# An attention and two gated layers on one core: the prologue before the first token block rebuilt

## The chip, the cores and the metric

The kernel runs on one core of a Trainium2 chip. TensorE (PE) multiplies matrices into PSUM, VectorE (DVE) and ScalarE (ACT) do elementwise work, GpSimd (POOL) does elementwise work on SBUF, SyncE (SP) issues most of the loads and stores. The engines run side by side and meet at semaphores. The metric is the time of one execution on the device in microseconds (us), and lower is better.

## What is computed

q, k and v have 6016 rows and 256 columns. The columns of q and k are normalised, their product is a 256 x 256 matrix of scores, its softmax is applied to v, and two token-wise layers follow.

```python
qn = q / (np.linalg.norm(q, axis=1, keepdims=True) + 1e-06)
kn = k / (np.linalg.norm(k, axis=1, keepdims=True) + 1e-06)
s = kn.transpose(0, 2, 1) @ qn / tau
a = np.exp(s - s.max(-1, keepdims=True))
a /= a.sum(-1, keepdims=True) + 1e-09
x = v @ a                                    # 6016 x 256
h = x @ w_in                                 # 6016 x 2048
P = a[0] + a[1] * h + a[2] * h**2 + a[3] * h**3
Q = 1.0 + np.abs(b[0]) * np.abs(h) + np.abs(b[1]) * h**2
y = (P / (Q + 1e-6)) @ w_out                 # 6016 x 256
out = (sigmoid(y @ w_gate) * (y @ w_val)) @ moe2_w_out   # hidden width 1536
```

In P, a is the input of four coefficients, elsewhere the softmax.

## The kernel before

**The prologue.** k and q come in 14 chunks of 1, 2, 4 x 10, 2 and 2 row tiles, through a ring of three buffers in `work` that SP fills (L277 to L285). PE adds each chunk's product into the scores (L658, fp32, two records for each 256-column product). ACT squares each chunk (L373, L376) and DVE adds the squares (L520). When all is added, DVE folds the sums (L509) and PE turns them into column norms (L665, L667). ACT takes the roots (L383, L384), DVE inverts them and scales the scores in two halves `c` (L526 to L536), finds the maximum of both halves in one instruction (L538) and negates it (L539). ACT takes the exponentials (L389), PE transposes them (L673), DVE copies the transposes to `att_t` (L545). PE then multiplies `att_t` by w_in into M, the product of softmax and w_in, in ten tiles in fp32 (`m_tile`, L648): four 256 columns wide ahead of block 0, the other six 512 wide, one in each of slots 0 to 5 of block 0. ACT and DVE split each tile into a high and a low part in fp32r (`split_m`, L363 and L486).

**Products in three.** All later products are of split operands, three fp32r matmuls for each (high by high, high by low, low by high; `product3`, L637 to L639, and `add_y`, L705 to L707). The weights are split too, in 13 chunks of 128 x 1024: ACT writes the high part (`weights_hi`, L351), POOL the low part (`weights_lo`, L327). Chunks 0 to 3 are w_out of the first layer, 4 to 9 the gate and value weights, 10 to 12 the last weights. Chunks 0 to 3 are split in the loads of k and q, 4 to 7 around the M tiles, 8 to 12 at the slots of the table `SPLIT`.

**The blocks.** The tokens are taken in 16 blocks of 376, each in 8 slots `j`, one slot for two of the 16 column tiles of h. In a slot PE multiplies v's block by M (`hidden`, twelve matmuls). ACT reads the result out of PSUM twice (L430, L433; the second signals `h_read`). DVE multiplies on (L598, L604: the Horner steps `horner1` and `horner2`), and both build the quotient P/Q by a seed and one Newton step: L448, L620 (`quad`), L462 (`seed`), then for the pair of the slot before L584, L588 (`scaled`), L414, L558 and L565 (`g`). Two slots later ACT splits the quotient's high part (L441) and POOL its low part (L339), and three slots later `add_y` multiplies it by w_out, twelve matmuls. PE's `hidden` waits for the slot before's L604 (`horner2`), since both use the same PSUM banks. The next token block's v is split by ACT and DVE (`split_v`, L357 and L480) at the head of its block, after the last `hidden` of the block before. The gate, value and last products of block 0 start in slot 3 of block 1, and from there on each slot has work of both layers.

Each engine runs its instructions in the order in which the code writes them. Names of code in what follows: `g_ready` is signalled by L565, `w_hi_ready` by L351, `w_lo_ready` by L327, `v_lo_ready` by L480, `norms_summed` by the norm matmuls.

Of the kernel before, what the change touches and what calls it, by code (L numbers as in the profile page):

```python
# [17 lines left out]
P = 128  # L18


def attention_rational_gated_kernel(nc, q, k, v, tau, w_in, w_out1, coef_a, coef_b, w_gate, w_val, w_out2, out):
# [39 lines left out]
    KQ_SPLIT = {4: 0, 6: 1, 8: 2, 10: 3}  # L61
    M_SPLIT = ((4, 5), (6, 7))
    KQ_SPLITS, READY = len(KQ_SPLIT), 8
    SPLIT = {(0, 0): 8, (0, 1): 9, (0, 6): 10, (0, 7): 11, (1, 0): 12}
    KQ_T = 4
    KQ_SIZES = [1, 2] + [KQ_T] * ((NT - 5) // KQ_T)
    KQ_SIZES += [2] * ((NT - sum(KQ_SIZES)) // 2) + [1] * ((NT - sum(KQ_SIZES)) % 2)
    KQ_CHUNKS = [(sum(KQ_SIZES[:n]), w) for n, w in enumerate(KQ_SIZES)]
    assert sum(KQ_SIZES) == NT and KQ_SIZES[-1] <= 2
    KQ_RING = 3  # L70

    with ExitStack() as ctx:
# [8 lines left out]
        w_stages = CC * C, 8 * TB  # L81
        with nc.sbuf_tensor("before", [P, 8 * TB + 8 * TB + CC * FF1], F32) as before:
            att_t = before[:, 0:CC * C].rearrange("p (a b) -> p a b", a=CC)
            early_stages = [before[:, at + n * W_CHUNK:at + (n + 1) * W_CHUNK]
                            for at in w_stages for n in range(2)]

            w_in_sb = [before[:, 16 * TB + d * FF1:16 * TB + (d + 1) * FF1] for d in range(CC)]
# [5 lines left out]
        w2_hi, w2_lo = sb("w2_hi", [P, T2, C], F32R), sb("w2_lo", [P, T2, C], F32R)  # L93


# [8 lines left out]
        KQ_W = KQ_T * C  # L104
        work = sb("work", [P, 10 * KQ_W])
# [15 lines left out]
        V_AT = 9 * PW  # L121
        v_in = region(V_AT, (CC, TB))
        STAGE_AT = V_AT + PW
        o_sb = region(STAGE_AT, (CC, TB))
        sg = [region(STAGE_AT + PW + n * TB, (TB,)) for n in range(2)]
        assert STAGE_AT + 2 * PW <= 10 * KQ_W
# [670 lines left out]
```

## Time and profile before

| | us |
|---|---|
| median of 3 runs | 1247.23 |
| the three runs | 1246.74 to 1249.14 |
| the profiled execution | 1247.94 |
| its span, first to last instruction | 1246.4 |
| first matmul of the scores | 4.63 |
| first `hidden` of block 0 | 66.25 |
| first `hidden` of slot 3 of block 1 | 158.50 |

The span is 1.5 us less than the profiled execution's own time, and that is 0.7 us above the median. In a row of the profile "ps<-v_hi,m_hi" means that the instruction writes `ps` and reads `v_hi` and `m_hi`; an arrow in brackets names what ended an engine's idle time. Matmul records overlap: one record of 0.33 us is followed 0.17 us later by the next where PE runs freely.

### The profile page before, as it was taken

How to read it: one execution, taken by the hardware profiler on the slowest of the kernel's cores; microseconds unless marked ns; L12 is line 12 of the kernel's file. 1: busy time of each engine (PE TensorE's matmuls, PEld its weight loads, DVE VectorE, ACT ScalarE, POOL GpSimd, SP SyncE). 2: the span in 40 equal slices, each digit the busy share in tenths (PEclk: the TensorE clock that was granted, in tenths of full speed). 3: DMA queues.
4: the chain of work that ended last, by engine and by line, in shares of the span. 5: the costliest groups of instructions: out<-in, count | busy, mean ns of one | idle time of the engine just before them, and what ended most of it. 6: DMA issues, size and time to landing. Idle time of an engine off the chain costs nothing.

```text
span 1246.4 us, 19492 instructions
## 1 busy us (share of the span) xinstructions
PE 1195.6 (96%) x6766; PEld 1175.9 (94%) x6766; DVE 1084.2 (87%) x1372; ACT 886.5 (71%) x1264; POOL 269.1 (22%) x150
## 2 busy tenths in 40 slices
PE   8768599999999999999999999999999999999998
PEld 6656599999999999999999999999999999999998
DVE  5779898989999998989999998989999998989842
ACT  5667577867777777867777777767777777767732
POOL 1252421212212222212212212212221212212210
PEclk9889799999999999999999999999999999999999
DMA  8820000000000000000000000000000000000000
GB/s 309 315 84 1 12 2 13 14 13 12 0 12 12 12 12 12 12 12 12 0 12 12 12 12 12 12 12 12 0 12 12 12 12 12 12 0 12 0 13 13
DMA packets 14708, 33.82 MB, mean 27 GB/s; under 512 B 1632, under 2 KB 5472, under 8 KB 14432
## 3 DMA queue, kind: packets, MB, share of 16 engines
q1 hardware_dynamic: 14256, 33.56, 7.7%
q8 instruction: 11, 0.18, 0.1%
q14 instruction: 9, 0.07, 0.0%
q10 hardware_dynamic: 432, 0.00, 0.0%
HBM read 27.40 MB, written 6.16 MB: 27 GB/s over the span
## 4 chain that ended last, share of the span: by engine, by line
PE 90%; DVE 5%; ACT 2%; issue 2%; DMA 1%; SPq 0%; DVEq 0%; ACTq 0%
PE ps L637 17%; PE ps L639 17%; PE ps L638 17%; PE ps L705 7%; PE ps L706 7%; PE ps L707 7%; PE ps L729 5%; PE ps L731 5%; PE ps L730 5%; PE ps L658 2%; DMA work<-in_q 1%; DVE work L620 1%; DVE work L598 1%; ACT work L433 1%; PE ps L648 1%
## 5 line engine op out<-in xcount | busy, mean ns | idle before, releaser
L339 POOL TENSOR_TENSOR g_parts<-work,g_parts 128x752 fp32r<-128x752 f32 x128 | 234.1, 1829 | 856.2 <-ACT g_parts L441 850.2
L430 ACT ACTIVATE work<-ps,neg_a 128x752 f32<-128x752 f32 x128 | 125.4, 979 | 155.7 <-PE ps L639 92.1
L637 PE MATMUL ps<-v_hi,m_hi 128*128 128x376 f32 x512 | 175.0, 342 | 31.5 <-DVE work L604 15.5
L639 PE MATMUL ps<-v_hi,m_lo 128*128 128x376 f32 x512 | 174.8, 341 | 0.0
L638 PE MATMUL ps<-v_lo,m_hi 128*128 128x376 f32 x512 | 173.8, 339 | 0.0
L705 PE MATMUL ps<-g_parts,w_hi 128*128 128x376 f32 x512 | 172.9, 338 | 0.0
L706 PE MATMUL ps<-g_parts,w_hi 128*128 128x376 f32 x512 | 170.9, 334 | 0.0
L707 PE MATMUL ps<-g_parts,w_lo 128*128 128x376 f32 x512 | 170.2, 332 | 0.0
L598 DVE TENSOR_TENSOR work<-work,ps 128x752 f32<-128x752 f32 x128 | 119.6, 934 | 47.3 <-ACT work L433 45.5
L462 ACT ACTIVATE work<-work,consts 128x752 f32<-128x752 int32 x128 | 117.6, 919 | 52.6 <-DVE work L620 52.6
L553 DVE TENSOR_TENSOR work<-work,ps 128x376 f32<-128x376 f32 x192 | 103.9, 541 | 52.6 <-PE ps L639 39.9
L414 ACT ACTIVATE work<-work,consts 128x752 f32<-128x752 f32 x128 | 118.3, 924 | 27.9 <-DVE work L584 27.9
L565 DVE SCALAR_TENSOR_TENSOR work<-work 128x752 f32<-128x752 f32 x128 | 122.2, 954 | 14.2
L637 PEld LDWEIGHTS ps<-v_hi,m_hi 128*128 128x128 f32 x512 | 98.4, 192 | 36.4 <-issue 14.2
L620 DVE TENSOR_TENSOR work<-work 128x752 f32<-128x752 f32 x128 | 132.2, 1032 | 0.0
L588 DVE SCALAR_TENSOR_TENSOR work<-work,neg_a 128x752 f32<-128x752 f32 x128 | 131.7, 1029 | 0.0
L409 ACT ACTIVATE ys<-work 128x376 fp32r<-128x376 f32 x192 | 98.9, 515 | 46.0 <-PE ps L731 45.9
L448 ACT ACTIVATE work<-work,abs_b 128x752 f32<-128x752 f32 x128 | 130.6, 1020 | 0.0
L604 DVE SCALAR_TENSOR_TENSOR work<-work,neg_a,ps 128x752 f32<-128x752 f32 x128 | 127.5, 996 | 2.9
L729 PE MATMUL ps<-ys,w_hi 128*128 128x376 f32 x384 | 129.1, 336 | 0.2 <-DVE ys L571 0.2
L637 PE MATMUL ps<-ys,wg_hi 128*128 128x376 f32 x384 | 127.9, 333 | 1.2 <-DVE ys L614 0.8
L639 PE MATMUL ps<-ys,wv_lo 128*128 128x376 f32 x384 | 128.7, 335 | 0.0
(94 smaller groups left out, 2869.2 us busy)
## 6 DMA issues: line engine op xcount, KB each, us to landing
work<-in_v SPq DMA_DIRECT2D x16, 376.0 KB, 3.0
out<-work SPq DMA_DIRECT2D x16, 376.0 KB, 2.3
work<-in_k SPq DMA_DIRECT2D x10, 512.0 KB, 4.7
work<-in_q SPq DMA_DIRECT2D x10, 512.0 KB, 6.1
before<-in_moe_w_out SPq DMA_DIRECT2D x6, 512.0 KB, 6.1
before<-in_moe_w_in SPq DMA_DIRECT2D x2, 1024.0 KB, 6.7
before<-in_moe_w_gate SPq DMA_DIRECT2D x3, 512.0 KB, 7.2
work<-in_moe_w_val SPq DMA_DIRECT2D x2, 512.0 KB, 10.1
```

The source lines that it names most:

```text
L339: nc.gpsimd.tensor_tensor(g_lo[n], g[n], as_f32(g_hi[n]), ALU.subtract).then_inc(g_lo_ready, 1)
L448: nc.scalar.activation(vb, ab, ACT.Identity, scale=abs_b[:, 1:2], bias=abs_b[:, 0:1]).then_inc(vb_ready, 1)
L588: nc.vector.scalar_tensor_tensor(out=poly[o], in0=poly[o], scalar=neg_a[:, 0:1], in1=seed[o], op0=ALU.add, op1=ALU.mult).then_inc(scaled, 1)
L598: nc.vector.tensor_tensor(poly[n], poly[n], ps_h, ALU.mult).then_inc(horner1, 1)
L620: nc.vector.tensor_tensor(quad[n], vb, ab, ALU.mult).then_inc(quad_ready, 1)
L637: nc.tensor.matmul(dst, l_hi, r_hi, start=(n == 0), stop=False)
L638: nc.tensor.matmul(dst, l_hi, r_lo, start=False, stop=False)
L639: last = nc.tensor.matmul(dst, l_lo, r_hi, start=False, stop=(n == len(parts) - 1))
L705: nc.tensor.matmul(acc_y[:, c, :], l_hi, r_hi, start=(j == 0 and x == 0), stop=False)
L706: nc.tensor.matmul(acc_y[:, c, :], l_hi, r_lo, start=False, stop=False)
L707: last = nc.tensor.matmul(acc_y[:, c, :], l_lo, r_hi, start=False, stop=(j == PAIRS - 1 and x == 1))
L729: nc.tensor.matmul(acc_o[:, c, :], l_hi, s_hi[n], start=(m == 0), stop=False)
```

## The change

It touches only what runs before block 1's slot 3, and the waits that go with it.

- **Two load queues.** The q half of the first four chunks is issued by ACT, the k half by SP. The small coefficient loads move behind chunk 3, and the DVE instructions on them behind chunk 6. The chunks are 1, 1, 2, 4 x 10 and 3 tiles, the ring has four buffers, in a place of its own (`kq`). v's block 0 is loaded after chunk 5, two of w_out's chunks after chunks 4 and 6, the other two and w_in (in eight pieces) behind the last chunk.
- **Norms amid the scores.** PE runs the norm matmuls ahead of the last chunk's products. ACT takes the q root first, then the k root, then splits w_out's chunks 2 and 3.
- **Softmax by halves.** For each half c: scores, minimum (of negated scores; the separate negation goes), exponential, transpose into a bank of its own, copy. `split_v(0)` moves ahead of the roots.
- **Block 0's y in fp32.** For block 0's pairs PE multiplies the unsplit quotient `g` by w_out as loaded (`w1_raw`): four fp32 matmuls (`add_raw_y`) instead of twelve fp32r ones, one slot earlier. ACT's and POOL's splits of `g` (L441, L339) fall away for these eight pairs.
- **Splits placed by slot.** Chunk 4's high part is done before block 0, those of 5 to 12 at the ends of slots 0 to 7; the low part of chunk 4 + n waits on POOL for `h_read` of slot n.
- **`split_v(1)`** moves from the head of block 1 to slot 7 of block 0.

```diff
+    KQ_SIZES = [1, 1, 2] + [4] * ((NT - 4) // 4) + [(NT - 4) % 4] * ((NT - 4) % 4 > 0)
+    KQ_RING = 4
+    V_AFTER, COEF_AFTER = 5, 3
+    W1_AFTER = {4: 0, 6: 1}
+    NORMS_BEFORE = len(KQ_CHUNKS) - 1
...
         def splits_v(i, first):
-            return first and not is_block(i, 0)
+            return first and not is_block(i, 0) and not is_block(i, 1)
...
+                if n >= KQ_RING:
+                    sp.dma_start(q_in[r][:, 0:w * C], q_v[:, t * C:(t + w) * C]).then_inc(kq_loaded[r], 16)
...
-            for n in range(READY):
+            for n in range(W1_CHUNKS):
                 weights_lo(n)
             def step(i, first, carry, head, tail):
                 for j, now, late, old, gone, early, second, left in slots(i, first, carry, head, tail):
-                    if old is not None:
+                    if isinstance(i, int) and i * PAIRS + j < len(chunks) - W1_CHUNKS:
+                        pool.wait_ge(h_read, now + 1)
+                        weights_lo(W1_CHUNKS + now)
+                    if old is not None and not unsplit(old):
...
+            split_v(0)
             act.wait_ge(consts_ready, 1)
             nc.scalar.activation(consts[:, 2:3], consts[:, 1:2], ACT.Sqrt, scale=-1.0)
             act.wait_ge(norms_summed, 1)
-            act.wait_ge(kq_multiplied, len(KQ_CHUNKS))
-            nc.scalar.activation(k_norm, ps_knorm, ACT.Sqrt)
             nc.scalar.activation(q_inv, ps_qnorm, ACT.Sqrt).then_inc(norms_rooted, 1)
+            nc.scalar.activation(k_norm, ps_knorm, ACT.Sqrt).then_inc(norms_rooted, 1)
+            for n in range(len(W1_AFTER), W1_CHUNKS):
+                weights_hi(n)
             nc.scalar.activation(consts[:, 3:4], consts[:, 1:2], ACT.Exp)
...
+            link(nc.vector.tensor_scalar(q_inv, q_inv, 1e-6, None, ALU.add))
+            link(nc.vector.reciprocal(q_inv, q_inv))
+            dve.wait_ge(norms_rooted, 2)
+            link(nc.vector.tensor_scalar(k_norm, k_norm, 1e-6, None, ALU.add))
             link(nc.vector.reciprocal(k_inv, k_norm))
             link(nc.vector.tensor_scalar(k_inv, k_inv, tau_inv, None, ALU.mult))
+            dve.wait_ge(kq_multiplied, len(KQ_CHUNKS))
             for c in range(CC):
                 link(nc.vector.scalar_tensor_tensor(out=att[:, c, :], in0=ps_kq[:, c, :], scalar=k_inv[:, c:c + 1],
                                                     in1=q_inv, op0=ALU.mult, op1=ALU.mult))
-            link(nc.vector.reduce_max(neg_max, att, AX_X))
-            nc.vector.tensor_scalar(neg_max, neg_max, -1.0, None, ALU.mult).then_inc(scores_ready, 1)
-            split_v(0)
+                nc.vector.tensor_reduce(neg_min[:, c:c + 1], att[:, c, :], AX_X, ALU.min).then_inc(scores_ready, 1)
+            for c in range(CC):
+                dve.wait_ge(att_turned, c + 1)
+                nc.vector.tensor_copy(att_t[:, :, c * P:(c + 1) * P], ps_attt[c]).then_inc(att_t_ready, 1)
...
+            def add_raw_y(pair):
+                j, n = pair % PAIRS, pair % 2
+                pe.wait_ge(g_ready, pair + 1)
+                for c in range(CC):
+                    for x in range(2):
+                        last = nc.tensor.matmul(acc_y[:, c, :], w1_raw[:, 2 * j + x, c * P:(c + 1) * P], g[n][:, x, :],
+                                                start=(j == 0 and x == 0), stop=(j == PAIRS - 1 and x == 1))
+                last.then_inc(y_added, 1)
...
+                    if old is not None and unsplit(old):
+                        add_raw_y(old)
```

ACT between the last squares and the first M tiles, before (L380 loads the roots' function table, L385 the exponential's, L391 the sigmoid's):

```order
L380 ACT_TABLE_LOAD
L380 ACTIVATE consts<-consts 128x1 [waits consts_ready]
L383 ACTIVATE small<-ps 128x2 [waits kq_multiplied,norms_summed]
L384 ACTIVATE work<-ps 128x256
L385 ACT_TABLE_LOAD
L385 ACTIVATE consts<-consts 128x1
L357 ACTIVATE v_hi<-work 128x752 [waits v_loaded]
L389 ACTIVATE work,small<-work,small 128x256 [waits scores_ready]
L389 ACTIVATE work,small<-work,small 128x256
```

The same place with the change (L366 is `weights_hi`):

```order
L372 ACTIVATE v_hi<-work 128x752 [waits v_loaded]
L401 ACT_TABLE_LOAD
L401 ACTIVATE consts<-consts 128x1 [waits consts_ready]
L403 ACTIVATE work<-ps 128x256 [waits norms_summed]
L404 ACTIVATE small<-ps 128x2
L366 ACTIVATE w_hi<-before 128x1024 [waits w_loaded2]
L366 ACTIVATE w_hi<-before 128x1024 [waits w_loaded3]
L407 ACT_TABLE_LOAD
L407 ACTIVATE consts<-consts 128x1
L410 ACTIVATE work,small<-work,small 128x256 [waits scores_ready] x2
```

Two weight splits now stand between the roots and the exponentials, POOL's low parts follow them, and the roots no longer wait for the last product of the scores.

POOL's splits in block 0, before:

```order
L339 TENSOR_TENSOR g_parts<-work,g_parts 128x752 [waits g_hi_ready] x2
L339 TENSOR_TENSOR g_parts<-work,g_parts 128x752 [waits y_added,g_hi_ready] x3
L327 TENSOR_TENSOR w_lo<-before,w_hi 128x1024 [waits w_hi_ready]
L339 TENSOR_TENSOR g_parts<-work,g_parts 128x752 [waits y_added,g_hi_ready]
L327 TENSOR_TENSOR w_lo<-before,w_hi 128x1024 [waits w_hi_ready]
```

And with the change:

```order
L338 TENSOR_TENSOR wg_lo<-before,wg_hi 128x2x512 [waits w_hi_ready,h_read]
L338 TENSOR_TENSOR wv_lo<-before,wv_hi 128x2x512 [waits w_hi_ready,h_read]
L338 TENSOR_TENSOR wg_lo<-before,wg_hi 128x2x512 [waits w_hi_ready,h_read]
L338 TENSOR_TENSOR wv_lo<-work,wv_hi 128x2x512 [waits w_hi_ready,h_read]
L338 TENSOR_TENSOR wg_lo<-work,wg_hi 128x2x512 [waits w_hi_ready,h_read]
```

Each slot has one weight split there now, and none of the quotient.

DVE at the end of block 0, before (from `horner2` of slot 7):

```order
L604 SCALAR_TENSOR_TENSOR work<-work,neg_a,ps 128x752 [waits horner1]
L620 TENSOR_TENSOR work<-work 128x752 [waits e2_ready,vb_ready]
L558 SCALAR_TENSOR_TENSOR work<-work 128x752 [waits scaled]
L565 SCALAR_TENSOR_TENSOR work<-work 128x752 [waits newton1,e2_ready]
L480 TENSOR_TENSOR v_lo<-work,v_hi 128x752 [waits v_hi_ready]
```

With the change:

```order
L621 SCALAR_TENSOR_TENSOR work<-work,neg_a,ps 128x752 [waits horner1]
L502 TENSOR_TENSOR v_lo<-work,v_hi 128x752 [waits v_hi_ready]
L639 TENSOR_TENSOR work<-work 128x752 [waits e2_ready,vb_ready]
L575 SCALAR_TENSOR_TENSOR work<-work 128x752 [waits scaled]
L582 SCALAR_TENSOR_TENSOR work<-work 128x752 [waits newton1,e2_ready]
```

The split of v's block 1 moved ahead of three instructions.

## Rows read from the trace of the kernel before

**Rows 1.** Busy time by stretches, then TensorE's granted clock, DMA share, GB/s.

```profile
130.00:140.00 10.00, 4.14 (x13) 4.14 (x14) 8.59 (x8) 3.51 (x4) 2.34 (x1) 0.50 0.14 39
...
160.00:200.00 40.00, 39.61 (x231) 39.23 (x230) 37.87 (x50) 30.64 (x44) 9.08 (x5) 1.00 0.00 1
...
300.00:1200.00 900.00, 900.00 (x5244) 899.73 (x5243) 818.43 (x1048) 663.42 (x957) 187.66 (x103) 1.00 0.03 10
```

**Rows 2.** Timeline (start, us, engine, line), slot 3 of block 1 on PE.

```profile
158.50 0.41 PE L637 MATMUL ps<-v_hi,m_hi 128*128 128x376 f32 x1 [1.95 <-DVE work L604]
```

**Rows 3.** Timeline, PE, the product of the scores, in stretches.

```profile
4.63 2.07 PE L658 MATMUL ps<-work 128*128 128x256 f32 x4 [4.63 <-DMA work<-in_q]
8.13 41.93 PE L658 MATMUL ps<-work 128*128 128x256 f32 x184 [1.42 <-DMA work<-in_q]
...
11.64 4.70 PE L658 MATMUL ps<-work 128*128 128x256 f32 x21
```

**Rows 4.** Timeline, from the norms to the maximum.

```profile
51.94 0.68 PE L667 MATMUL ps<-work,ones 128*128 128x256 f32 x2
...
52.72 0.38 ACT L384 ACTIVATE work<-ps 128x256 f32<-128x256 f32 x1
...
53.46 1.75 DVE L530 RECIPROCAL work<-work 128x256 f32<-128x256 f32 x1
...
55.53 1.00 DVE L536 SCALAR_TENSOR_TENSOR work<-ps,small,work 128x256 f32<-128x256 f32 x2
56.57 0.69 DVE L538 TENSOR_REDUCE small<-work 128x2 f32<-128x512 f32 x1
```

**Rows 5.** Timeline, from the exponentials to block 0.

```profile
57.50 0.51 ACT L389 ACTIVATE work<-work,small 128x256 f32<-128x256 f32 x1 [2.17 <-DVE small L539]
...
59.37 0.69 DVE L545 COPY before<-ps 128x512 f32<-128x512 f32 x1 [0.37 <-PE ps L673]
...
60.11 6.49 PE L648 MATMUL ps<-before 128*128 128x256 f32 x16 [0.78 <-DVE before L545]
...
66.25 0.52 PE L637 MATMUL ps<-v_hi,m_hi 128*128 128x376 f32 x1
```

**Rows 6.** Weight splits on POOL (a group, one alone), two DVE instructions beside such splits.

```profile
L327 POOL TENSOR_TENSOR wg_lo<-before,wg_hi 128x1024 fp32r<-128x1024 f32 x3 | 7.0, 2349 | 18.8 <-ACT wg_hi L351 18.8
...
83.69 2.98 POOL L327 TENSOR_TENSOR wv_lo<-work,wv_hi 128x1024 fp32r<-128x1024 f32 x1 [4.57 <-ACT wv_hi L351]
...
84.38 3.09 DVE L588 SCALAR_TENSOR_TENSOR work<-work,neg_a 128x752 f32<-128x752 f32 x1
...
133.34 2.46 DVE L480 TENSOR_TENSOR v_lo<-work,v_hi 128x752 fp32r<-128x752 f32 x1 [0.75 <-ACT v_hi L357]
```

**Rows 7.** Timeline, POOL and then DVE in slot 4 of block 0.

```profile
104.22 1.80 POOL L339 TENSOR_TENSOR g_parts<-work,g_parts 128x752 fp32r<-128x752 f32 x1 [5.84 <-ACT g_parts L441]
...
103.86 1.00 DVE L604 SCALAR_TENSOR_TENSOR work<-work,neg_a,ps 128x752 f32<-128x752 f32 x1
104.77 0.74 DVE L486 SCALAR_TENSOR_TENSOR m_lo<-ps,small,m_hi 128x512 fp32r<-128x512 f32 x1
105.43 1.39 DVE L620 TENSOR_TENSOR work<-work 128x752 f32<-128x752 f32 x1
106.74 0.93 DVE L558 SCALAR_TENSOR_TENSOR work<-work 128x752 f32<-128x752 f32 x1
...
111.49 1.00 DVE L604 SCALAR_TENSOR_TENSOR work<-work,neg_a,ps 128x752 f32<-128x752 f32 x1
```

**Rows 8.** ACT: the second read of h in slot 5, and the weights' high parts (a group).

```profile
109.70 0.79 ACT L433 ACTIVATE work<-ps 128x752 f32<-128x752 f32 x1
...
L351 ACT ACTIVATE w_hi<-before 128x1024 fp32r<-128x1024 f32 x6 | 6.3, 1042 | 0.0
```

**Rows 9.** Timeline, PE: an M tile of 512 columns, and slot 0 of block 1.

```profile
76.33 1.88 PE L648 MATMUL ps<-before 128*128 128x512 f32 x4
...
135.86 0.68 PE L637 MATMUL ps<-v_hi,m_hi 128*128 128x376 f32 x1 [10.57 <-DVE v_lo L480]
```

More of the change, by code:

```diff
@@ L103, in attention_rational_gated_kernel @@
         PW = 2 * TB
[L104 to L105 removed]
+        STAGE_AT = 10 * PW
+        work = sb("work", [P, STAGE_AT + 2 * W_CHUNK])
         def region(at, shape):
@@ L228, in is_block, with unsplit @@
             return isinstance(i, int) and i == n
+        def unsplit(pair):
+            return isinstance(pair, int) and pair < PAIRS
         def splits_v(i, first):
-            return first and not is_block(i, 0)
+            return first and not is_block(i, 0) and not is_block(i, 1)
         def steps(eng, step):
@@ L396, in _ @@
                 split_m(n)
-            for n in M_SPLIT[1]:
-                weights_hi(n)
+            weights_hi(W1_CHUNKS)
             act.wait_ge(coefs_ready, 1)
@@ L435, in step @@
                         split_m(M_FIRST + j)
-                    if old is not None:
+                    if is_block(i, 0) and j == PAIRS - 1:
+                        split_v(1)
+                    if old is not None and not unsplit(old):
                         act.wait_ge(g_ready, old + 1)
+                        if is_block(i, 1):
+                            act.wait_ge(y_added, PAIRS)
+                            act.wait_ge(w_lo_ready, len(chunks))
                         wait_count(act, y_added, old + (-1))
-                        if is_block(i, 0) and j == 2:
-                            act.wait_ge(w_lo_ready, READY)
                         nc.scalar.activation(g_hi[n], g[n], ACT.Copy).then_inc(g_hi_ready, 1)
@@ L460, in step @@
                         act.wait_ge(quad_ready, now + 1)
-                        wait_count(act, g_lo_ready, now + (-1))
+                        if unsplit(now) or (is_block(i, 1) and j < 2):
+                            wait_count(act, y_added, now + (-1))
+                        else:
+                            act.wait_ge(g_lo_ready, now + (-1))
                         nc.scalar.activation(seed[n], quad[n].bitcast(I32), ACT.Sigmoid, scale=SEED_SCALE,
@@ L525, in _ @@
-            dve.wait_ge(norms_rooted, 1)
-            nc.vector.tensor_scalar(q_inv, q_inv, 1e-6, None, ALU.add).then_inc(small_step, 1)
-            nc.vector.tensor_scalar(k_norm, k_norm, 1e-6, None, ALU.add).then_inc(small_step, 1)
-            done[0] += 2
-            dve.wait_ge(small_step, done[0] - 1)
-            nc.vector.reciprocal(q_inv, q_inv).then_inc(small_step, 1)
-            dve.wait_ge(small_step, done[0])
-            done[0] += 1
+                if n == COEF_AFTER + 3:
+                    constants()
@@ L611, in step @@
                         split_m(M_FIRST + j)
+                    if is_block(i, 0) and j == PAIRS - 1:
+                        split_v(1)
                     if j == 2 and head:
@@ L755, in step @@
                         gate_and_value(*early)
-                    if gone is not None:
+                    if gone is not None and not unsplit(gone):
                         add_y((j - 3) % PAIRS, gone, i)
```

196 lines of the change are left out of this document (98 added, 98 removed).

## The prediction, made before the changed kernel ran

> **What bounds the kernel now.** I read the stretches first. From 160 us on PE is busy all the time at full clock (900.00 of 900 us between 300 and 1200) [rows 1], so from there the time is PE's work, which the change leaves as it is. Ahead of that PE waits: of the ten us from 130 on it works 4.14, at the lower clock level (granted 0.50, 1.2 GHz). The timeline shows where this ends: `hidden` of slot 3 of block 1 starts at 158.50 after a wait for DVE's L604 [rows 2], and from there PE runs on. From that start to the end both kernels do the same work. So the question is only when that start comes, and the gain is its shift.
>
> Before it lie three stages: the scores, from 4.63 [rows 3] to the end of the norms at 51.94 + 0.68 = 52.62 [rows 4], the softmax and M up to 66.25 [rows 5], and eleven slots, 158.50 - 66.25 = 92.25 us.
>
> **The scores.** PE has 188 records of 256 columns. 184 of them take 41.93 us from 8.13 [rows 3]: 8 at the lower clock at 0.43 and 176 at 0.216 make 41.4, so PE bounds this stage and the loads cost 0.5. (21 records from 11.64 in 4.70, the last end included, agree.) In front of them stand four records from 4.63 and a wait of 1.42 for chunk 1's load [rows 3]. With the change chunk 1 is half as large and loads from two queues, so I take the first record at 4.2 (bounds 3.8 and 4.6) and no wait. The clock will rise as PE has been busy a while; before, that was after 12 records, and I keep 12: 4.2 + 12 x 0.43 = 9.4. The norms now come after 176 records: 164 x 0.216 = 35.4, so 44.8, and 0.8 for the norm matmuls themselves (L667's 0.68 and a little for L665): norms at 45.6, 7.0 earlier. Of that, 2.6 is the last chunk (12 x 0.216), which PE now multiplies while ACT and DVE work on the roots. Bounds: 0.9 either way for four records more or fewer at the lower clock, and up to 1 more if chunks 4 to 6, which now share the loads with v and two chunks of w_out, come late. The sums of the last squares must be ready by 44.8: its loads are issued when chunk 9 is done, 10.4 us earlier, which leaves about 1 us; this I count at nothing.
>
> **Norms to scores.** Before: 55.53 - 52.62 = 2.9 us, of which L530 is 1.75 [rows 4]. Now the k root no longer stands ahead (-0.1), but its addition and two small instructions come behind the reciprocal (+0.4): 3.2, to 48.8. At that time the scores' last product (to 48.1) is ready. Here I expect a new wait. ACT now splits two w_out chunks behind the roots, and POOL follows. In the trace DVE instructions without a PSUM operand stand still while POOL subtracts: L588 at 84.38 takes 3.09, to 0.8 after the end of POOL's 83.69 + 2.98 = 86.67; L480 takes 2.46 [rows 6]. Those with a PSUM operand don't: L604 and L486 keep 1.00 and 0.74 beside POOL's L339 [rows 7]. No row shows a one-input SBUF instruction beside POOL. It costs nothing if it goes free like L486, and up to all of POOL's time if it waits like L588; being without PSUM operand, it is nearer to L588, and I take the wait. With N the norms' end, ACT's first split (1.04 [rows 8]) ends at N + 1.5, POOL's (2.35 [rows 6]) at N + 3.9; the k addition, due at N + 2.55, waits for it, POOL's second split goes in behind it until N + 6.5, and the multiplication by 1/tau waits for that. Scores start at N + 6.8 = 52.4 instead of 48.8: 3.6 lost, with bounds 0 and 4.8 (the reciprocal too waits, or POOL behind it).
>
> On this the Trainium skill ("SBUF — State Buffer", Who interferes with whom) says that a DVE instruction with at most one SBUF input, outside the 2-port modes, does not contend with GpSimd, but that `tensor_scalar` can run in a 2-port mode and then does. By the first half the sum would be the first rival below; by the second the addition and the multiplication wait and the sum is the forecast's. That two-input instructions wait, the trace agrees.
>
> **Softmax and M.** Before, from the scores to the M tiles 60.11 - 55.53 = 4.6 [rows 4, 5]. By halves: score 0.5, minimum 0.45 (L538's 0.69 is for both halves; bounds 0.35 and 0.69), then the second half's 0.9 on DVE beside the first exponential; the second exponential and its read-out 0.6, its transposes 0.5. M starts at +3.1 behind them, since the first copy (half of L545) is done by then. The M tiles took 66.25 - 60.11 = 6.1, nearly all at the lower clock; 16 records cost 3.5 at full clock, 6.9 at half. PE's pause before them is still 4 us and more, so some stay slow: 5.1. Block 0 starts at 52.4 + 3.1 + 5.1 = 60.6, 5.7 earlier. ACT's sigmoid table and row sums end before the first M tile does.
>
> **The slots.** Take slot 4 to 5 [rows 7]: L604 to L604 is 111.49 - 103.86 = 7.63, and DVE never pauses in it. L620 is 1.31 of that, because POOL's split of `g` runs until 106.02; alone it would take 0.93 as L558 does and hand on 0.07 before its end, 0.86. Without POOL's `g` split a slot is 7.2 with an M tile and 6.5 without (L486 is 0.66). POOL's weight split now starts at `h_read`. In the old slot 5 that is 109.70 + 0.79 = 110.5 [rows 8], just as DVE reaches the PSUM-reading L598, L604 and L486, together 2.55; the split is 2.35. So it fits with an M tile, and costs L620 0.6 without. DVE stays the bound: from L604's end, hidden (12 x 0.17), both reads (1.7) and handover are 4.0, less than DVE's 5.2; ACT's weight split (0.95) ends as the quotient does, at 3.4, and costs nothing while the margin of about 0.1 holds. L604 ends at 5.9 after block 0's start (hidden, two reads, two Horner steps), then 7.0 (slot 1, where ACT's split does delay), 5 x 7.2, 7.1 (slot 7), 9.8 (slot 8: v's split 0.9 + 0.6 of wait, and two quotients), 6.2 and 6.5: 78.5. The old slot 8 alone cost 10.57 of PE's waiting for v [rows 9]; most of that goes.
>
> PE's own part: an M tile's record is 0.43 for 512 columns [rows 9], so an fp32 record of 376 is 0.32 (bounds 0.31 by columns, 0.43 uncut), and a pair's eight make 2.5 instead of twelve at 0.17, 2.05. Slot: 2.05 + 1.7 + 2.5 = 6.3 of 7.2, under DVE. Where PE idles, the clock falls to 1.2 GHz in the rows [rows 1]; I expect it behind slot 0 (0.5), at slots 1 to 2 (0.7), slot 9 (1.3) and slot 3 of block 1 (1.7, since slot 2 of block 1 no longer has a y product and PE pauses 4 us): 4.3 together, bounds 1 and 7. Eleven slots: 82.8 instead of 92.25, 9.4 saved.
>
> **The sum.** 5.7 + 9.4 = 15.1. The profiled execution took 1247.94, so 1232.8; it lay 0.7 above the median, so 1232.1 as a median.
>
> **Rivals.**
> - *No wait for POOL in the softmax* (one-input instructions go free). For it: no row shows such a one waiting. 3.6 better: 1228.5.
> - *POOL gets in front of L588 in some slots.* POOL starts when `h_read` comes before DVE has begun L588; then L588 waits as at 84.38, 2.1 us each [rows 6]. By my times `h_read` comes 0.8 after L588 starts. In two to four slots it makes 1236 to 1241.
> - *The same in all nine slots with a weight split*: 9 x 2.1 = 18.9, 1251, slower than before. It decides if ACT runs over 0.8 us ahead, which needs `g_ready` not to hold its first read; the order of the waits speaks against it.
> - *PE bounds block 0 at the lower clock*: a slot of 12.5 us there. A PE so busy has been raised to full clock each time in this trace; if the rise comes a few us late in two or three slots, 1238.
> - *Better still*: with the first rival and little time at the lower clock, 1225.
>
> **The numbers.** Forecast 0.45; softmax without wait 0.26; POOL ahead in a few slots 0.13; PE late 0.05; better still 0.05; POOL ahead in all slots 0.04; no effect 0.02. A measurement can tell 0.2%, 2.5 us, from no change. Range 1225 to 1240, leaving out the far ends of the second to fourth rivals and of the last. Faster 0.94, same 0.02, slower 0.04. Predicted: 1232.1.
>
> **What would show it.** The norms' matmuls at about 45; the k addition and the multiplication by 1/tau on DVE each beginning or ending with a POOL split (or, for the first rival, lasting 0.2); block 0 at 60.6; DVE's slots at 7.2 without a long L588; PE without its wait at block 1's head; `hidden` of block 1's slot 3 at 143 to 144, and after it a PE as full as before. Wrong it would be if PE waits for chunks between 10 and 25 us, if a long L605 (the old L588) stands in the slots, or if PE's records in block 0 stay at half clock.

## The result, and the profile after

The changed kernel takes 1233.47 us (median of 4 runs, 1232.38 to 1234.48), the one before in the same comparison 1247.50 (1246.74 to 1249.14): a ratio of 0.9886, 95% interval 0.9869 to 0.9903. It was forecast as 1232.1 within 1225 to 1240. The profiled execution took 1234.48 us with a span of 1232.7, so the span fell by 13.7. In a timeline each row gives start, duration, engine, line, what it writes and reads, and in brackets the idle time ahead and what ended it.

The scores and the norms on PE, timeline of the changed kernel (to be held against [rows 3, 4]; L690 is the product, L678 and L680 the norms):

```profile
3.87 3.78 PE L690 MATMUL ps<-kq 128*128 128x256 f32 x8 [3.87 <-DMA kq<-in_k]
8.53 1.99 PE L690 MATMUL ps<-kq 128*128 128x256 f32 x8 [0.89 <-DMA kq<-in_k]
11.05 14.39 PE L690 MATMUL ps<-kq 128*128 128x256 f32 x64 [0.52 <-DMA kq<-in_q]
25.71 20.99 PE L690 MATMUL ps<-kq 128*128 128x256 f32 x96 [0.28 <-DMA kq<-in_q]
47.16 0.58 PE L678 MATMUL ps<-ones,work 128*128 128x1 f32 x4 [0.46 <-DVE work L541]
47.60 0.68 PE L680 MATMUL ps<-work,ones 128*128 128x256 f32 x2
48.12 2.75 PE L690 MATMUL ps<-kq 128*128 128x256 f32 x12
```

The norms end at 48.28 instead of 52.62 [rows 4]: 4.3 us earlier, not the 7.0 of the forecast. PE waited four times for a chunk of k or q (0.89, 0.52, 0.28, and 0.45 at 21.7, inside the third row) and 0.46 for DVE's folds. The first eight records stand 0.43 us apart, those behind 8.53 at 0.22; the granted clock reads 1.00 here all the time, in both kernels, so that the lower clock of the first records is read from their spacing alone.

From the norms to block 0, the same view, several engines (L546 to L551 invert the norms, L554 the scores, L669 the M tiles; the rows are in order of engine):

```profile
49.78 4.65 POOL L338 TENSOR_TENSOR w_lo<-before,w_hi 128x1024 fp32r<-128x1024 f32 x2 [18.36 <-ACT w_hi L366]
...
49.06 1.75 DVE L547 RECIPROCAL work<-work 128x256 f32<-128x256 f32 x1
50.85 1.31 DVE L549 TENSOR_SCALAR small<-small 128x2 f32<-128x2 f32 x1
52.19 0.17 DVE L550 RECIPROCAL small<-small 128x2 f32<-128x2 f32 x1
52.39 2.06 DVE L551 TENSOR_SCALAR small<-small 128x2 f32<-128x2 f32 x1
54.49 0.48 DVE L554 SCALAR_TENSOR_TENSOR work<-ps,small,work 128x256 f32<-128x256 f32 x1
...
57.45 6.28 PE L669 MATMUL ps<-before 128*128 128x256 f32 x16
63.38 0.52 PE L656 MATMUL ps<-v_hi,m_hi 128*128 128x376 f32 x1
```

The addition L549 works on two numbers in each partition and takes 1.31 us, to 52.16; the multiplication L551 takes 2.06, to 54.45. POOL's two splits run from 49.78 to 54.43, 2.3 each. The two reciprocals, one of them wholly inside POOL's second split, do not wait: L547, more than half of it beside POOL, keeps the 1.75 that it has before [rows 4], and L550 takes 0.17. Block 0 starts at 63.38, 2.9 earlier than before [rows 5].

A slot of block 0 (slot 2), POOL, then DVE (to be held against [rows 7]; L639 is the old L620):

```profile
82.43 2.37 POOL L338 TENSOR_TENSOR wg_lo<-before,wg_hi 128x1024 fp32r<-128x1024 f32 x1 [4.81 <-ACT work L451]
...
82.38 0.94 DVE L615 TENSOR_TENSOR work<-work,ps 128x752 f32<-128x752 f32 x1
83.36 1.00 DVE L621 SCALAR_TENSOR_TENSOR work<-work,neg_a,ps 128x752 f32<-128x752 f32 x1
84.27 0.74 DVE L508 SCALAR_TENSOR_TENSOR m_lo<-ps,small,m_hi 128x512 fp32r<-128x512 f32 x1
84.93 0.93 DVE L639 TENSOR_TENSOR work<-work 128x752 f32<-128x752 f32 x1
```

POOL's split fills the time in which DVE reads PSUM, and L639 has 0.93 where L620 had 1.39. L621 starts at 68.54, 76.18, 83.36, 90.53, 97.71, 104.89, 112.06, 118.97, 128.63, 135.44 and 141.96. PE's waits between 43 and 150 us (in total, times, longest):

```profile
PE ps L656 <- DVE work L621: 10.8, 5, 4.3
PE ps L699 <- ACT work L410: 5.3, 1, 5.3
PE ps L656 <- DVE m_lo L508: 5.1, 3, 2.7
PE ps L656 <- DVE v_lo L502: 2.2, 1, 2.2
```

The wait for v's block 1 was 10.57 [rows 9] and is 2.2. `hidden` of block 1's slot 3 starts at 143.10 and not at 158.50 [rows 2], 15.4 earlier. Its row in the timeline:

```profile
143.10 0.65 PE L656 MATMUL ps<-v_hi,m_hi 128*128 128x376 f32 x1 [4.29 <-DVE work L621]
```

The span fell by 13.7, so 1.7 was lost behind that point. The stretches show where (length, busy time of PE, its weight loads, DVE, ACT and POOL, then the granted clock):

```profile
130.00:140.00 10.00, 8.47 (x32) 6.32 (x30) 8.00 (x10) 6.05 (x7) 0.00 (x0) 0.83 0.00 0
140.00:146.00 6.00, 2.90 (x9) 2.93 (x10) 5.54 (x7) 4.95 (x7) 1.78 (x1) 0.60 0.00 0
146.00:160.00 14.00, 14.00 (x77) 14.00 (x77) 12.76 (x17) 10.29 (x17) 3.43 (x2) 0.93 0.01 2
300.00:1200.00 900.00, 899.17 (x5238) 898.59 (x5237) 809.80 (x1040) 657.82 (x952) 184.38 (x102) 1.00 0.03 10
```

### The profile page after: what moved, and what is told of

Read it like the earlier page. It is cut to its first block, busy times and chain, and to the rows that moved or that the text cites. A ratio compares the mean times of both kernels' runs of the same rounds, so it can differ in the third digit from the quotient of the medians.

```text
span 1232.7 us, 19435 instructions
## 1 busy us (share of the span) xinstructions
PE 1196.4 (97%) x6734; PEld 1167.0 (95%) x6734; DVE 1078.6 (88%) x1374; ACT 881.1 (71%) x1256; POOL 251.1 (20%) x144
## 4 chain that ended last, share of the span: by engine, by line
PE 89%; DVE 5%; ACT 2%; DMA 1%; issue 1%; SPq 0%; ACTq 0%; DVEq 0%
PE ps L658 18%; PE ps L656 18%; PE ps L657 17%; PE ps L728 7%; PE ps L729 7%; PE ps L730 7%; PE ps L762 5%; PE ps L764 5%; PE ps L763 5%; DMA kq<-in_q 1%; DVE work L534 1%; DVE work L582 1%; DVE work L615 1%; ACT work L448 1%; DVE work L575 1%
## 5 line engine op out<-in xcount | busy, mean ns | idle before, releaser
L353 POOL TENSOR_TENSOR g_parts<-work,g_parts 128x752 fp32r<-128x752 f32 x120 | 218.7, 1822 | 831.6 <-ACT g_parts L462 831.6
L728 PE MATMUL ps<-g_parts,w_hi 128*128 128x376 f32 x480 | 160.6, 334 | 0.0
L729 PE MATMUL ps<-g_parts,w_hi 128*128 128x376 f32 x480 | 160.0, 333 | 0.0
L730 PE MATMUL ps<-g_parts,w_lo 128*128 128x376 f32 x480 | 159.4, 332 | 0.0
L621 DVE SCALAR_TENSOR_TENSOR work<-work,neg_a,ps 128x752 f32<-128x752 f32 x128 | 127.4, 995 | 2.9
L639 DVE TENSOR_TENSOR work<-work 128x752 f32<-128x752 f32 x128 | 128.9, 1007 | 0.0
L658 PE MATMUL ps<-ys,wg_lo 128*128 128x376 f32 x384 | 128.7, 335 | 0.0
L764 PE MATMUL ps<-ys,w_lo 128*128 128x376 f32 x384 | 128.5, 335 | 0.0
```

What stands on the lines that cost most here:

```text
L353: nc.gpsimd.tensor_tensor(g_lo[n], g[n], as_f32(g_hi[n]), ALU.subtract).then_inc(g_lo_ready, 1)
L658: last = nc.tensor.matmul(dst, l_lo, r_hi, start=False, stop=(n == len(parts) - 1))
L728: nc.tensor.matmul(acc_y[:, c, :], l_hi, r_hi, start=(j == 0 and x == 0), stop=False)
L729: nc.tensor.matmul(acc_y[:, c, :], l_hi, r_lo, start=False, stop=False)
L730: last = nc.tensor.matmul(acc_y[:, c, :], l_lo, r_hi, start=False, stop=(j == PAIRS - 1 and x == 1))
L764: last = nc.tensor.matmul(acc_o[:, c, :], l_lo, s_hi[n], start=False, stop=(m == T2 - 1))
```

## The experiments

All start from the changed kernel, `s5_w1_late` and `s10_best` from it by way of `s1_pool_late`. Differences in time are to its 0.9886 or its 1233.47, or to the 0.9874 and 1233.90 of its second comparison (`s11_after`, below). The kernel before ran beside each comparison and had medians from 1247.50 to 1249.11, so a difference of medians and one of ratios can disagree by 1.6 us; where it matters, both are given. A row of the profile is from one execution, and the unchanged prologue differs by about 1 us from one to the next (`s11_after`).

### Who lengthens L549 and L551

Theory: POOL. `s1_pool_late` moves POOL's two low parts out of the softmax.

```diff
             for n in range(W1_CHUNKS):
+                if n == 2:
+                    pool.wait_ge(row_inv_ready, 1)
                 weights_lo(n)
```

> POOL's low parts of w_out's chunks 2 and 3 wait until the row sums are inverted; nothing else changes, ACT's high parts stay where they are. Theory (DVE's one-input instructions wait for POOL): L549 falls from 1.31 us to about 0.16 and L551 from 2.06 to about 0.2, as the reciprocal beside them (0.17), the scores start 3.0 us earlier, near 51.5, and the time is about 3 us less than with the change alone, near 1230.5. Rival 1 (these two are slow for another reason, such as waiting for each other's result): both stay at 1.3 and 2.1 and the time is the same. Rival 2 (the gain is given back): POOL's two splits now run beside the M tiles and the first slot, something waits there instead, the scores start 3 us earlier but the first hidden less than 2 us earlier.

Measured: 1229.87 us, ratio 0.9845 (0.9831 to 0.9858), span 1226.6. Its timeline, DVE, PE and POOL (L551 and L553 are the old L549 and L551, L671 the M tiles):

```profile
50.85 0.17 DVE L551 TENSOR_SCALAR small<-small 128x2 f32<-128x2 f32 x1
51.05 0.17 DVE L552 RECIPROCAL small<-small 128x2 f32<-128x2 f32 x1
51.25 0.23 DVE L553 TENSOR_SCALAR small<-small 128x2 f32<-128x2 f32 x1
51.51 0.48 DVE L556 SCALAR_TENSOR_TENSOR work<-ps,small,work 128x256 f32<-128x256 f32 x1
...
54.26 3.62 PE L671 MATMUL ps<-before 128*128 128x256 f32 x16
55.24 4.71 POOL L338 TENSOR_TENSOR w_lo<-before,w_hi 128x1024 fp32r<-128x1024 f32 x2 [23.87 <-DVE small L564]
57.53 0.53 PE L658 MATMUL ps<-v_hi,m_hi 128*128 128x376 f32 x1
```

The cause is shown: with nothing else moved both fall to about 0.2, and the scores start 2.98 earlier (51.51 for 54.49). In `s5_w1_late`, where POOL's splits fall beside them again, they take 1.32 and 2.07. This is what the prediction took over its first rival. The Trainium skill ("SBUF — State Buffer", Who interferes with whom) says that `tensor_scalar` can enter a 2-port mode, and that then whichever of VectorE and GpSimd issues first keeps the shared ports for its whole instruction and the other is blocked; the traces agree, also for instructions of two elements (1.31 and 2.06 us behind a split that POOL had begun, 0.17 and 0.23 without it).

But the first `hidden` came 5.85 earlier, not 3. The other 2.7 is in the M tiles: 16 records in 3.62 us, where the changed kernel needs 6.28. PE's pause ahead of the transposes was 5.34 and is 2.36, and the granted clock from 46 to 66 us is 1.00 for 0.83. The theory had left that out; the next runs test it. The profiled execution was one of the two fastest of its five; in the medians the run is 3.6 us below the changed kernel, by the ratios 5.1.

### What the lower clock costs

`s7_warm_m` fills PE's pause ahead of the transposes.

```diff
+            for _ in range(20):
+                nc.tensor.matmul(ps[:, 4, 0:C], ones[:], q_acc[:, 0, :], start=True, stop=True)
             pe.wait_ge(ident_ready, 1)
```

> 20 matmuls of 256 columns that nobody reads (4.3 us at full clock) fill PE's pause between the last product of the scores and the transposes; the results stay as they are. Theory (the pause costs PE its clock for the M tiles): the granted clock stays at full through the M tiles, their 16 records take 3.6 us as in s1_pool_late instead of 6.28, the first hidden starts 2.3 to 2.7 us earlier, near 60.9, and as much of it stays to the end as the later dips of the clock leave: 1231 to 1232. Rival (M's tiles are paced by the splits on ACT and DVE or by w_in's load, and the clock only looks like the cause): the M tiles take over 5 us, no change.

Measured: 1234.17 us, ratio 0.9879 (0.9862 to 0.9897). The M tiles ran at full clock, 3.72 us, but began at 60.76 and not at 57.4. I had counted one record for an fp32 matmul, and there are two:

```profile
51.23 8.80 PE L696 MATMUL ps<-work,ones 128*128 128x256 f32 x40
60.76 3.72 PE L669 MATMUL ps<-before 128*128 128x256 f32 x16 [0.30 <-DVE before L559]
```

So gain and delay cancelled: the median is 0.7 higher than the changed kernel's, by the ratios 0.9 lower. `s9_warm_m10` has 10 instead of 20.

> As s7_warm_m, but 10 added matmuls instead of 20: in s7_warm_m each left two records of 0.22 us, so that the 20 took 8.80 us and ran 3.3 us past the point at which the M tiles could have started; the M tiles themselves took 3.72 us as the theory said. With 10 (4.4 us, 50.9 to 55.3) nothing is delayed. Theory: M tiles from 57.4 in 3.7 us, first hidden near 60.8, 2.6 us earlier than the changed kernel's, time 1231 to 1232.5 (less than 2.6 if the lower clock then falls on slot 1 or 2). Rival: the M tiles take over 5 us again, time as the changed kernel's.

Measured: 1230.93 us, ratio 0.9859 (0.9844 to 0.9874); the changed kernel on the same chip 1233.90.

```profile
50.96 4.48 PE L696 MATMUL ps<-work,ones 128*128 128x256 f32 x20
...
57.52 3.62 PE L669 MATMUL ps<-before 128*128 128x256 f32 x16
60.78 0.52 PE L656 MATMUL ps<-v_hi,m_hi 128*128 128x376 f32 x1
```

The M tiles begin at 57.52, where the changed kernel has 57.45, and the first `hidden` is at 60.78, 2.6 earlier than its 63.38. The clock alone cost that; splits and loads did not pace the M tiles. From the start of the M tiles to the first `hidden` is 3.26 us here and 4.92 to 5.93 in six profiles of the unchanged prologue, so the clock costs 1.7 to 2.7 there, and the changed kernel's own profile is the costliest. The median is 3.0 lower, by the ratios 1.9, and their intervals overlap.

`s8_warm_slots` does the same in slot 2 of block 1.

```diff
+    WARM = {(1, 2): 20}
...
+                    for _ in range(WARM.get((i, j), 0) if isinstance(i, int) else 0):
+                        nc.tensor.matmul(ps_gate, m_hi[:, 0, 0:P], v_hi[:, 0, :], start=True, stop=True)
```

> 20 matmuls of 376 columns that nobody reads (3.4 us at full clock) fill PE's pause in slot 2 of block 1; the results stay as they are. Theory (the lower clock from slot 3 of block 1 on costs what the shift of 15.4 us to that slot lost to the end, 1.7 us): the granted clock is 1.00 from 140 to 160, PE works as much there as 14 us before at full clock, time 1.7 us less, near 1231.8. Rival 1 (it costs nothing, since DVE's chain holds the next slot anyway): the clock is 1.00 and the time the same. Rival 2 (the added matmuls delay hidden of slot 3): later by up to 1 us.

Measured: 1231.79 us, ratio 0.9867 (0.9850 to 0.9885), span 1229.8. The stretch of 140 to 146 us and the next, columns as above:

```profile
140.00:146.00 6.00, 5.17 (x31) 4.88 (x30) 5.52 (x7) 3.92 (x6) 1.80 (x1) 1.00 0.02 4
146.00:160.00 14.00, 13.62 (x79) 13.25 (x78) 13.60 (x18) 12.21 (x18) 3.65 (x2) 1.00 0.00 1
```

L622 (the old L621) of slot 2 of block 1 starts at 140.64, 1.32 ahead of 141.96, for reasons that lie before the added matmuls; the span is 2.9 shorter. The difference, 1.6, is what the full clock gives behind that point: the 1.7 that the result had lost. From that start to the end of the span is 1089.2 us here, 1089.1 in the kernel before (from its L604 at 157.35) and 1090.7 in the changed kernel's profile; in `s11_after`, the same code, it is 1090.0, so an execution loses 0.8 to 1.6 there.

`s11_after` is the changed kernel again.

> The changed kernel once more, to stand beside the other two on the same chip: 1233.5, with the first hidden between 62.6 and 63.4 as the clock rises sooner or later in the M tiles, which was seen in the profiles of s4_pool_free, s6_g_dummy and s8_warm_slots, whose code up to there is the same.

Measured: 1233.90 us (1231.06 to 1235.89), ratio 0.9874 (0.9856 to 0.9891); first `hidden` at 62.93, M tiles in 6.13. The place at which the clock rises and falls differs from one profile to the next where the code is the same: M tiles 6.28, 6.13, 5.62, 5.54, 5.33 and 5.27 us, first `hidden` from 62.41 (`s3_v_head`) to 63.38, and slot 1 (L621 to L621) took 7.64 in the first profile and 6.97 here. But here slot 2 took 8.55 for 7.18 and slot 9 7.56 for 6.81: the loss moved and did not go. The Trainium skill ("TensorE: Matmul & The Clock Gate", What's actually happening) says that the number of slow matmuls varies from run to run of one kernel; these traces agree.

### What paces the slots

`s4_pool_free` takes POOL's wait for `h_read` away.

```diff
                     if isinstance(i, int) and i * PAIRS + j < len(chunks) - W1_CHUNKS:
-                        pool.wait_ge(h_read, now + 1)
                         weights_lo(W1_CHUNKS + now)
```

> POOL's weight splits in block 0 no longer wait for h_read, only for the high part. Theory (a split that comes before L605 stops it until the split ends): POOL starts at about 80.6 in slot 2 instead of 82.4, L605 takes 2 to 3 us instead of 0.99, a slot takes 1.4 to 2.1 us more in seven or eight slots, time 1244 to 1250. Rival (in the slots DVE has slack that takes the wait up, or the engines share evenly): L605 stays below 1.5 us, the slots stay at 7.2 and the time is that of the changed kernel, near 1233.5; a small gain is possible since L639 of slots 6 and 8 would go free (0.4 each).

Measured: 1246.36 us, ratio 0.9982 (0.9973 to 0.9991). Its slot 2 on POOL and DVE (L604 is the L605 of the changed kernel and the L588 of [rows 6]):

```profile
79.46 2.99 POOL L338 TENSOR_TENSOR wg_lo<-before,wg_hi 128x1024 fp32r<-128x1024 f32 x1 [3.89 <-ACT wg_hi L365]
...
80.15 3.10 DVE L604 SCALAR_TENSOR_TENSOR work<-work,neg_a 128x752 f32<-128x752 f32 x1
83.17 0.92 DVE L614 TENSOR_TENSOR work<-work,ps 128x752 f32<-128x752 f32 x1
```

L604 takes 3.10, as L588 did once before the change (3.09 [rows 6]). A slot with an M tile takes 9.16 for 7.18. Without this one wait 12 of the 14 us are gone (by the ratios). It is the prediction's third rival, set off: L604 takes 3.1 in seven slots, 2 to 8, each 2.1 too long as forecast, and the slots lose 2.0 with an M tile and 1.6 to 1.7 without. The rival had counted nine slots and 18.9 us; slot 0 has no L604, and in slot 1 it stays at 1.00.

`s6_g_dummy` gives POOL one more subtraction in slots 2 to 7.

```diff
                         pool.wait_ge(h_read, now + 1)
+                        if is_block(i, 0) and old is not None:
+                            pool.wait_ge(g_ready, old + 1)
+                            nc.gpsimd.tensor_tensor(scratch[:], g[j % 2], g[j % 2], ALU.subtract).then_inc(dummy, 1)
                         weights_lo(W1_CHUNKS + now)
...
+                        if is_block(i, 0) and j >= 2:
+                            act.wait_ge(dummy, j - 1)
```

> POOL gets back one 128x752 subtraction in each of slots 2 to 7 of block 0, as the split of the quotient was, ahead of its weight split (it writes to a buffer that nobody reads; the results of the kernel are the same). Theory (the gain in the slots came from POOL having less to do beside DVE): POOL is then busy for 4.2 us from h_read on, DVE's three PSUM readers take 2.6 of them, L639 waits for the rest, 1.6 to 1.7 us, in six slots: about 10 us, time near 1243. Rival (only the new order of POOL's splits matters, and a DVE instruction shares rather than waits): 0.4 us for each slot, 2.5 in all, 1236.

Measured: 1239.57 us, ratio 0.9928 (0.9913 to 0.9943), 5.2 more than the changed kernel by the ratios and 6.1 in the median: between theory and rival.

```profile
80.96 1.44 POOL L352 TENSOR_TENSOR scratch<-work 128x752 f32<-128x752 f32 x1 [4.81 <-ACT work L456]
...
82.36 2.39 POOL L340 TENSOR_TENSOR wg_lo<-before,wg_hi 128x1024 fp32r<-128x1024 f32 x1
...
83.46 2.08 DVE L646 TENSOR_TENSOR work<-work 128x752 f32<-128x752 f32 x1
```

The mechanism is the theory's: DVE's L646 (old L639) waits until POOL is done at 84.75 and ends 0.8 later. The size was not: the added instruction took 1.44, not the 1.80 of the real split [rows 7], so L646 lost 1.15 in a slot. Taking the split of `g` off POOL was thus worth more than the 0.45 a slot of the prediction, given that the weight split stands in the same place.

`s3_v_head` puts v's split back to the head of block 1.

```diff
-            return first and not is_block(i, 0) and not is_block(i, 1)
+            return first and not is_block(i, 0)
...
-                    if is_block(i, 0) and j == PAIRS - 1:
-                        split_v(1)
```

> The split of v's block 1 goes back from slot 7 of block 0 to the head of block 1, all else as in the changed kernel. Theory (DVE and ACT, not PE, set the pace there): hidden of block 1's slot 0 starts at about 125.5 instead of 121.3, since v's split then follows the quotient of slot 7 and ACT's last weight split, but L621 of that slot, now at 128.63, is only 1 to 2.5 us later, because in the changed kernel two quotients and the wait for seed already held DVE; time 1235 to 1236. Rival (the whole of PE's wait is on the path): hidden and L621 both 4 us later, 1237.5. Second rival (v's split costs DVE the same 0.9 us wherever it stands, and PE's wait is hidden): no change, 1233.5.

Measured: 1235.55 us, ratio 0.9899 (0.9880 to 0.9917). PE's wait for it, in the list of waits:

```profile
PE ps L652 <- DVE v_lo L500: 5.8, 1, 5.8
```

The wait grew by 3.6 (2.2 before). The Horner step L619 of slots 7, 8 and 9 stands at 117.72, 130.44 and 136.52: 12.72 and 6.08, where the changed kernel has 9.66 and 6.81. (130.44 alone is 1.8 behind the 128.63 of the changed kernel, since slot 7 stood 1.25 ahead of it for reasons before the edit.) So 3.1 of the 3.6 reach slot 8's step, more than the theory's 1 to 2.5 and less than the rival's 4, and 0.7 comes back in slot 9, which is as short here as `s10_best` has it at full clock (6.12). Net 2.3 later in the trace, 2.1 in the median and 1.6 by the ratios, whose intervals (0.9880 to 0.9917, and 0.9869 to 0.9903 for the changed kernel) overlap. The time is the theory's; that most of PE's wait is hidden is not shown.

### What the scores wait for

`s2_norms_last` moves the norms behind the last chunk.

```diff
-                if n == NORMS_BEFORE:
-                    norms()
...
                 last.then_inc(kq_multiplied, 1)
+            norms()
```

> The norms go behind the last chunk's products, all else as in the changed kernel. Theory (PE bounds the scores, so the last chunk stood ahead of the norms): the norm matmuls end at about 50.1 instead of 48.3 (12 records of 0.216 us less the 0.46 that PE waited for the folds), everything behind them is 1.8 to 2.2 us later, time near 1235.5. Rival (the norms wait for DVE's folds anyway, or the wait for POOL absorbs the shift): the scores start within 0.5 us of 54.5 and the time is that of the changed kernel.

Measured: 1235.42 us, ratio 0.9893 (0.9878 to 0.9908). The norms end at 50.24 and the scores start at 56.45, both 1.96 later, as expected, and the M tiles 1.95 later (59.40). L621 of slot 1 is at 76.79: only 0.6 later than in the profile of the changed kernel, where slot 1 fell into the lower clock, but 1.7 later than in that of `s11_after` (75.06), where it did not. By slot 2 it is 0.6 and 0.4 later (83.97 for 83.36 and 83.61). The median is 2.0 higher, by the ratios 0.9, with intervals that overlap. So the shift of the scores is shown, and how much of it reaches the end is not.

`s5_w1_late` builds on `s1_pool_late` and takes w_out's loads out of the scores.

```diff
-    W1_AFTER = {4: 0, 6: 1}
+    W1_AFTER = {}
```

> On top of s1_pool_late: w_out's chunks 0 and 1 are loaded behind the last chunk of k and q and their high parts stand with those of 2 and 3 behind the roots; POOL's four low parts wait for the row sums. Theory (PE's late chunks in the scores came from loads that share the DMA engines): the waits of 0.5, 0.45 and 0.28 us at 11, 21.7 and 25.7 us go, the waits at 8.5 and perhaps 11 stay, since nothing but k and q is on the way then; the norms start 0.7 to 1.2 us earlier, near 46.2. Rival (the chain of squares and sums on ACT and DVE, back to back from 30 us on, sets the norms): the norms start within 0.3 of 47.2 although the waits go. Behind the norms ACT has 2 us more to do before the exponentials, of which 1.5 to 2 delays them, so the time is 0 to 1.5 us more than s1_pool_late's, and POOL's four splits reach to 65, into slot 0.

Measured: 1231.64 us, ratio 0.9862 (0.9844 to 0.9880). One thing I had written wrongly: POOL's wait stood at its third chunk, so its first two low parts, now late, fell into the softmax again and lengthened the two small instructions (1.32 and 2.07). For the scores the run still answers:

```profile
8.43 38.25 PE L692 MATMUL ps<-kq 128*128 128x256 f32 x168 [0.79 <-DMA kq<-in_k]
46.52 0.50 PE L680 MATMUL ps<-ones,work 128*128 128x1 f32 x4
```

From 8.43 on PE waits for no load and not for the folds, and the norms start at 46.52 instead of 47.16. But that the waits are gone is not due to w_out: `s3_v_head` and `s6_g_dummy`, with the loads of the changed kernel, have none behind 8.4 either, and their norms start at 47.15 and 47.18. What these three share is a slow start of PE behind that wait. Stretches of PE (length, busy time, clock, DMA share, GB/s), of the changed kernel and then of this run:

```profile
8.45:10.45 2.00, 1.92 (x8) 1.00 0.95 369
...
8.45:10.45 2.00, 2.00 (x5) 1.00 1.02 404
```

Eight records begin in the one and five in the other. Where PE is quick behind the wait it waits for chunks afterwards, where it is slow the chunks are there, and the norms start at nearly the same time. So I read PE and the loads as about equally near to the bound, which is argued and not tested. (In `s4_pool_free`, up to there the same code, PE also waits 1.34 for DVE's folds.) Without w_out's two chunks they start 0.6 earlier. That is the cost of these loads with their splits, since ACT's two high parts and POOL's two low parts left the scores with them. The chunks of k land in 5.1 us (median) with the ring of four as it is, for 6.9 in the changed kernel and 4.7 before with the ring of three, so the depth of the ring does not explain the 6.9. The rest of the 2.7 us by which the norms are later than forecast stays unexplained in its parts. In time the run is 1.8 above `s1_pool_late` (2.1 by the ratios), where 0 to 1.5 was expected.

### All of it together

`s10_best` is `s1_pool_late` with filler matmuls in PE's pauses (as in `s8_warm_slots`, but into bank 0 in slots 0 and 1 of block 0, and with `m_hi` as both operands in its slot 7).

```diff
+    WARM = {(0, 0): 10, (0, 1): 16, (0, 7): 8, (1, 0): 12, (1, 1): 8, (1, 2): 20}
...
+                if n == 2:
+                    pool.wait_ge(row_inv_ready, 1)
...
+            for _ in range(4):
+                nc.tensor.matmul(ps[:, 4, 0:C], ones[:], q_acc[:, 0, :], start=True, stop=True)
```

> s1_pool_late with matmuls that nobody reads in PE's pauses: 4 ahead of the transposes, 10, 16 and 8 in slots 0, 1 and 7 of block 0, 12, 8 and 20 in slots 0, 1 and 2 of block 1; the results stay as they are. In s1_pool_late the clock still fell in slots 2, 9 and 11. Theory: it stays at full in all of 50 to 160 us; slot 2 gains 0.4 us, slot 9 gains 0.9 to 1.3, slot 3 of block 1 gains 0.9 to 1.7: together 2.2 to 3.4 less than s1_pool_late, near 1227. Rival 1: DVE's chain paces these slots, so a full clock gains under 1 us, 1229. Rival 2: the added matmuls hold up hidden in a slot or two, up to 1 us each, 1229 to 1231.

Measured: 1225.71 us (1225.00 to 1226.11, 5 runs), ratio to the kernel before 0.9812 (0.9799 to 0.9825); the changed kernel on the same chip 1233.90. Its stretch of 50 to 150 us, columns as above:

```profile
50.00:150.00 100.00, 89.67 (x404) 69.98 (x404) 89.22 (x110) 76.60 (x99) 30.27 (x14) 1.00 0.16 51
```

The same stretch of the changed kernel:

```profile
50.00:150.00 100.00, 74.79 (x272) 53.78 (x271) 85.01 (x100) 70.62 (x90) 28.03 (x13) 0.90 0.16 52
```

The clock is full throughout. Against `s1_pool_late` the Horner step of slot 2 comes 7.19 after slot 1's (7.59), that of slot 9 6.12 after slot 8's (7.63); slot 3 of block 1 gains nothing (8.37 for 8.38), and 0.7 comes behind slot 2 of block 1 (1089.2 us to the end for 1089.9). Together the span is 2.6 shorter than in `s1_pool_late`. It is the fastest version, 8.2 us below the changed kernel and 23.4 below the one before (1249.11 in that comparison).

## Why the prediction held, step by step

| step | predicted | measured |
|---|---|---|
| first record of the scores | 4.2 | 3.87 |
| 176 records before the norms | 40.6 | 40.7 |
| waits for chunks, for the folds | 0, 0 | 2.14, 0.46 |
| norm matmuls; their end | 0.8; 45.6 | 1.12; 48.28 |
| norms to scores | 6.8 | 6.21 |
| scores to M tiles | 3.1 | 2.96 |
| M tiles to block 0 | 5.1 | 5.93 |
| block 0 starts | 60.6 | 63.38 |
| to slot 3 of block 1, and clock lost behind it | 82.8 in all | 79.7 + 1.7 |
| saved in all | 15.1 | 13.7 |

- **The scores: mis-sized by 2.7 us.** The norms moved ahead as said (`s2_norms_last`: 1.96 later without that), but PE is not the only bound, as the prediction had it: "no wait" for chunks was wrong, and so was "at nothing" for the last sums. The bound of 1 us for late chunks was too small: with two queues the first record starts sooner (3.87 for 4.63), but later chunks still come late. The prediction had named PE waiting between 10 and 25 us as what would make it wrong; it did wait there, 1.0 us, so one of its own signs of being wrong came true.
- **Norms to scores: right, mechanism and size.** The port wait was taken at 3.6, bounds 0 and 4.8; `s1_pool_late` gives 2.98. That the reciprocals go free was part of the choice, and they do. The analogy behind the choice (no PSUM operand, so it waits) does not hold in full: the reciprocals have none either.
- **M tiles: the clock is the term.** 0.8 too little in this profile, but 5.1 lies within the 4.92 to 5.93 that the same code takes from one execution to the next. A full clock was worth up to 2.7 here (`s9_warm_m10`), and the prediction had not asked how much of it could be had back.
- **The slots: right in form.** 7.18 for 7.2, 6.91 for 7.1, 9.66 for 9.8. L639 lost 0.4 and 0.3 in slots 6 and 8 (1.32 and 1.22 for 0.93), where 0.6 was forecast. The clock losses were put at 4.3. In this profile they are 0.7 in slot 1 (7.64 against 6.97 in `s11_after`), 0.7 in slot 9 (6.81 against 6.12 in `s10_best`) and 1.6 behind slot 2 of block 1 (`s8_warm_slots`), 3.0; in `s11_after` 1.4 in slot 2, 1.4 in slot 9 and 0.8 behind, 3.6.
- **The sum.** The scores' 2.7 and the M tiles' 0.8 too little, less 0.6 and 0.1 in the softmax and 1.4 in the slots: 1.4 us, the difference between 15.1 and 13.7. The errors partly cancel, and that is luck: the closeness of 1232.1 to 1233.47 is better than the steps.
- **The rivals.** No wait for POOL: refuted by `s1_pool_late`. Its price, 3.6 by the forecast, measured 3.6 in the medians and 5.1 by the ratios, since the clock adds to the 3.0 of the two instructions. POOL in front of L605: not so in any slot, but only because of `h_read`; `s4_pool_free` shows the 2.1 us on that instruction that was forecast and all but loses the gain. PE late at the lower clock: in one slot, 0.7 (1.4 in `s11_after`).

Not tested: the softmax by halves and the second load queue each alone, and block 0's y in fp32 apart from what it takes off POOL.

## What to carry to other kernels

Ahead of moving GpSimd work into a "free" place, look at which VectorE instructions run there: in these traces those that read PSUM went free, the reciprocals too, and small one-input additions on SBUF waited as long as large two-input ones. Put such work behind the signal after which VectorE reads PSUM, and say in the code why. Where TensorE pauses for some microseconds ahead of a chain that others wait for, look at the granted clock behind the pause: filler matmuls that ended before the work came cost nothing (ten gained 2.6 us at the first `hidden`), and too many cost what they gained (twenty).

## What the runs showed of the hardware that I had not expected

- A VectorE addition on 128x2 numbers took 1.31 us and a multiplication 2.06, each to the end of the GpSimd instruction beside it, while a reciprocal on the same 128x2 numbers took 0.17 in the same stretch.
- A shorter pause of TensorE (2.36 us for 5.34) brought the 16 records behind it to full clock (3.62 us for 6.28), so that removing a 3 us wait on VectorE gave 5.85 us at the first `hidden`.
- An fp32 matmul of 256 columns leaves two records of 0.22 us: 20 took 8.80 us.
